# Strassen's scheme for the second product of both MLP layers, on weights split once and fetched back

## The reference, cut to what matters

```python
gate = 1.0 / (1.0 + np.exp(-(x @ w_gate)))      # layer 1, 512 -> 1536
x = (gate * (x @ w_val)) @ w_out                # 1536 -> 512
h = x @ w_in                                    # layer 2, 512 -> 2048
x = (h * (1.0 / (1.0 + np.exp(-1.702 * h)))) @ w_out2   # 2048 -> 512
```

## Time and profile before

| | us |
|---|---|
| median of 3 runs | 897.64 (897.04 to 898.20) |
| profiled execution, own time | 896.92 |
| its span | 895.2 |
| PE busy | 887.3 |
| POOL busy | 694.8 |
| ACT busy | 483.5 |
| DVE busy | 472.2 |
| granted TensorE clock | 1.000 |

### The profile page before, as it was taken

How to read it: one execution, slowest core, us unless ns; L and a number is a source line. 1 busy time by engine, 2 the same in 40 slices (tenths; PEclk the granted TensorE clock), 3 DMA queues, 4 the chain that set the end, 5 groups by cost and what they waited for, 6 DMA issues and landing times.

```text
span 895.2 us, 17338 instructions
## 1 busy us (share of the span) xinstructions
PE 887.3 (99%) x6572; PEld 831.2 (93%) x6572; DVE 472.2 (53%) x865; ACT 483.5 (54%) x967; POOL 694.8 (78%) x551
## 2 busy tenths in 40 slices
PE   8999999999999999999999999999999999999998
PEld 6878899999999999999898899999998999989897
DVE  5767545555555455554544455555545445454545
ACT  5777755554445455545555455544645554545542
POOL 6679989998779999758787869998757887566551
PEclk9999999999999999999999999999999999999999
DMA  9776112222221222222221222422222212132111
GB/s 333 251 226 219 54 62 71 71 69 74 69 67 55 71 72 71 71 71 71 71 71 52 67 72 70 141 72 71 71 72 68 74 48 93 50 120 92 48 48 70
DMA packets 26722, 80.38 MB, mean 90 GB/s; under 512 B 2960, under 2 KB 3216, under 8 KB 26640
## 3 DMA queue, kind: packets, MB, share of 16 engines
q1 hardware_dynamic: 26640, 79.28, 27.5%
HBM read 74.55 MB, written 4.72 MB: 89 GB/s over the span
## 4 chain that ended last, share of the span: by engine, by line
PE 98%; DMA 1%; SPq 1%; issue 0%; DVE 0%
PE o_ps L432 39%; PE d_ps L442 7%; PE d_ps L445 7%; PE d_ps L444 7%; PE s_ps L442 6%; PE s_ps L445 6%; PE s_ps L444 6%; PE t_ps L442 3%; PE t_ps L445 3%; PE t_ps L444 3%; PE o_ps L405 1%; PE o_ps L425 1%; PE t_ps L376 1%; PE t_ps L417 1%; PE s_ps L330 1%; PE t_ps L390 1%
## 5 line engine op out<-in xcount | busy, mean ns | idle before, releaser
L1271 DVE TENSOR_TENSOR att<-o_ps,att 128x512 f32<-128x512 f32 (+1 forms) x245 | 152.4, 626 | 150.5 <-PE o_ps L432 150.5
L1518 POOL TENSOR_TENSOR w_lo<-w_sum,w_hi 128x1024 fp32r<-128x1024 f32 x60 | 144.1, 2402 | 66.0 <-ACT w_hi L782 66.0
L1513 POOL TENSOR_TENSOR w_lo<-w_raw,w_hi 128x768 fp32r<-128x768 f32 x60 | 111.0, 1849 | 44.1 <-ACT w_hi L778 44.1
L442 PE MATMUL d_ps<-xs_hi,w_hi 128*128 128x384 f32 x360 | 120.5, 335 | 0.0
L445 PE MATMUL d_ps<-xs_hi,w_lo 128*128 128x384 f32 x360 | 120.4, 335 | 0.0
L444 PE MATMUL d_ps<-xs_lo,w_hi 128*128 128x384 f32 x360 | 120.4, 334 | 0.0
L1531 POOL TENSOR_TENSOR v_lo<-v_raw,v_hi 128x1024 fp32r<-128x1024 f32 x42 | 100.7, 2398 | 20.3 <-ACT v_hi L786 20.3
L432 PE MATMUL o_ps<-v_hi,g_hi 128*128 128x512 f32 x288 | 111.9, 389 | 0.8 <-DVE att L1271 0.8
L432 PE MATMUL o_ps<-v_hi,g_lo 128*128 128x512 f32 x288 | 112.3, 390 | 0.0
L432 PE MATMUL o_ps<-v_lo,g_hi 128*128 128x512 f32 x288 | 112.3, 390 | 0.0
L1492 POOL TENSOR_TENSOR w_sum<-w_raw 128x256 f32<-128x256 f32 x120 | 88.4, 736 | 23.6 <-PE t_ps L445 20.2
(11 more groups left out here) (135 smaller groups left out, 1993.6 us busy)
## 6 DMA issues: line engine op xcount, KB each, us to landing
v_raw<-in_w_out_dram SPq DMA_DIRECT2D x42, 512.0 KB, 3.5
w_raw<-in_w_gate_val_dram SPq DMA_DIRECT2D x36, 512.0 KB, 3.6
w_raw<-in_w_in_dram SPq DMA_DIRECT2D x24, 512.0 KB, 3.5
vw<-in_v_win_dram SPq DMA_DIRECT2D x16, 390.0 KB, 4.9
vt<-in_v_tok_dram SPq DMA_DIRECT2D x16, 320.0 KB, 3.8
qk<-in_q_t_dram SPq DMA_DIRECT2D x16, 288.0 KB, 3.5
qk<-in_k_t_dram SPq DMA_DIRECT2D x16, 288.0 KB, 4.5
out_dram<-att SPq DMA_DIRECT2D x17, 256.0 KB, 4.5
```

The lines of the kernel that those rows point to most:

```text
L442: pe.matmul(bank, wh[:, w, cols], xh[:, x, c, :], start=(start and c == 0), stop=False, skip_group_check=True)
L1271: vec.tensor_tensor(part, value, part, ALU.add).then_inc(y_added, 1)
L1513: gp.tensor_tensor(w_lo[b % 2][:, A11:A22 + 1, :], w_raw[b % 2][:, R11:R22 + 1, :], w_hi[b % 2][:, A11:A22 + 1, :], ALU.subtract).then_inc ...
L1518: gp.tensor_tensor(w_lo[b % 2][:, S1:S4 + 1, :], w_sum[b % 2][:, S1:S4 + 1, :], w_hi[b % 2][:, S1:S4 + 1, :], ALU.subtract).then_inc(ws_re ...
```

## The change

It changes all of the MLP but the first phase's group order and the arithmetic of the first product.

- Phases are (1,0), (1,1), (1,2), (2,0), (2,1), (2,2). Phase 0 keeps the plain second product. The other 36 groups go in 18 pairs c, c+1 (n is c+2, the next pair's first group). A pair's second product is Strassen's too, in both layers feature-major: 7 tiles of 2 outputs of 12 matmuls of 384 columns (`second_pair`, order in TILES). Activations get their own sums T1 to T4, made in PSUM by VectorE (make_t1 to make_t4), copied by ScalarE (save11, save21, save12, hi_t1 to hi_t4) and split.
- Output weights of a pair are split into 7 pieces by `split_pair` on GpSimd and v_a12 to v_a22 on ScalarE, 11 and 7 operations of 128x512. They have one buffer, whose slots come free as the tiles end (`v_free`). Their raw weights are loaded by `load_pair` into one buffer.
- Input weights are split once. Layer 1's twelve blocks are stored to DRAM in phase 0 (`spill`, 1.83 MB each), layer 2's eight are made as jobs 0 to 7 in phases 0 to 2 in unused x slots (`job_sums`, `job_lows`, `job_a`, `job_s`, `store_job`). From phase 1 on each block is fetched back in three transfers: five of seven pieces (1.31 MB) behind the fifth product of the block that had the slot (`fetch_12`), then one behind its sixth and one behind its seventh (`fetch_3`).
- x has 10 slots (`ring`) in place of 14: B11, B21, T2 of the next phase are made early, T1, T3, T4, B22 when the last block's products free their slots (`late_x`). With c+2 the first group of a phase, `late_x` stands on GpSimd ahead of `split_pair(c + 2)`.
- In layer 1's pairs ScalarE's list ends v_a12(n), hi_t4(d), v_s1(n), v_a11(n), the activations of n, v_s2(n), v_s4(n), v_s3(n). For the first pair v_a12, v_s1, v_a11 stand ahead of snap_u2 of the pair's last block and v_s2, v_s4, v_s3, v_a22 ahead of save11, hi11 and snap_u3. ScalarE's job_a and job_s stand ahead of snap_u2(FIRST[d]) or, for jobs 2, 4 and 7, of snap_u2(FIRST[n]).
- VectorE's list of pair_of_two ends: add 9, add 10, low11(n), add 11, c22(n), add 12, add 13, low22(n).
- The output leaves feature-major, one store per pass and eight of 192 KB at the end; the host transposes it.

The parts of the diff that the text speaks of (SP, PE, ACT, POOL in this order):

```diff
-OB1, OB2 = 2 * KC, 2 * NT // P
-PHASES = [(1, 0), (1, 1), (2, 0), (1, 2), (2, 1), (2, 2)]
+OB1 = 2 * KC
+PHASES = [(1, 0), (1, 1), (1, 2), (2, 0), (2, 1), (2, 2)]
...
+JOBS = G2
+JOB_AT = (7, 7, 4, 4, 4, 1, 1, 1)
+JOBS_BEFORE = (0, 2, 5, 8)
...
+TILES = ((VA12, B21, True, 0, 0), (VS1, T1, True, 1, 1), (VS4, B22, False, 0, 1), (VA11, B11, True, 0, 0),
+         (VS2, T2, False, 0, 1), (VS3, T3, False, 1, 1), (VA22, T4, False, 1, 0))
+OBP = 2 * NP
+SINCE = (8, 6, 10, 6, 4, 8, 14)
+G_OUT = {g: 2 * i + 2 for i, (v, g, start, r, t) in enumerate(TILES)}
+V_OUT = {v: 2 * i + 2 for i, (v, g, start, r, t) in enumerate(TILES)}
...
+def v_free(c, piece):
+    return y_count(c) if c == G1 else y_count(c - 2) + V_OUT[piece]
...
+            def fetch_12(b):
+                if b >= NB:
+                    return
+                if b < MADE + 2:
+                    sp.wait_ge(spilled[b % 2], 16 * (MADE // 2))
+                if b == FIRST[NL1]:
+                    sp.wait_ge(job_stored, 16 * JOBS)
+                sp.wait_ge(in_done[b % 2], count(b - 2, 5))
+                sp.dma_start(w[b % 2][:, :, A11:S3 + 1, :].bitcast(F32), w_split[split_at(b), :, :, A11:S3 + 1, :]).then_inc(w_in1[b % 2], 16)
+            def fetch_3(b):
+                if b >= NB:
+                    return
+                sp.wait_ge(in_done[b % 2], count(b - 2, 6))
+                sp.dma_start(w[b % 2][:, :, A22, :].bitcast(F32), w_split[split_at(b), :, :, A22, :]).then_inc(w_in3[b % 2], 16)
+                sp.wait_ge(in_done[b % 2], count(b - 2, 7))
+                sp.dma_start(w[b % 2][:, :, S4, :].bitcast(F32), w_split[split_at(b), :, :, S4, :]).then_inc(w_in4[b % 2], 16)
+            def load_pair(c):
+                if c >= NG:
+                    return
+                if c == G1:
+                    sp.wait_ge(wa_ready, MADE)
+                    sp.wait_ge(wsum_ready, MADE)
+                else:
+                    sp.wait_ge(vp_ready, NP * pair(c))
+                q, lay, p, g = GROUPS[c]
+                source = w_out1 if lay == 1 else w_out2
+                for i in range(2):
+                    sp.dma_start(raw[:, i, :, :].rearrange("p a n -> p (a n)"), source[g + i]).then_inc(vp_loaded, 16)
...
+            def store_job(j):
+                sp.wait_ge(job_lo, 2 * j + 2)
+                sp.dma_start(w_split[MADE + j], job_w[JOB_AT[j]][:, :, :, :].bitcast(F32)).then_inc(job_stored, 16)
...
+            for c in range(G1, NL1, 2):
+                steps = range(LAST[c] if c > G1 else FIRST[c + 1], FIRST[c + 2] + 1)
+                if c == G1:
+                    load_job(2)
+                if c == G1 + 6:
+                    load_job(5)
+                for b in steps:
+                    fetch_3(b + 1)
+                    fetch_12(b + 2)
+                    if b == FIRST[c + 1]:
+                        load_pair(c + 2)
+                    if c in (G1 + 2, G1 + 8) and b == FIRST[c + 1]:
+                        store_job(3 if c == G1 + 2 else 6)
+                        load_job(4 if c == G1 + 2 else 7)
+                if c in (G1, G1 + 6):
+                    store_job(2 if c == G1 else 5)
+                    load_job(3 if c == G1 else 6)
+                if c in (G1 + 2, G1 + 8):
+                    store_job(4 if c == G1 + 2 else 7)
+            for c in range(NL1, NG - 2, 2):
+                for b in (FIRST[c + 1], FIRST[c + 2]):
+                    fetch_3(b + 1)
+                    fetch_12(b + 2)
+                load_pair(c + 2)
...
+            def second_pair(c, i):
+                v_part, g_part, start, r, t = TILES[i]
+                pe.wait_ge(vp_ready, NP * pair(c) + V_LOWS[v_part])
+                if g_part in t_ready:
+                    pe.wait_ge(t_ready[g_part], strassen(c + 1))
                 else:
-                    s = o % (OB2 // 2)
-                    toks = slice(s * P, (s + 1) * P)
-                    passes(bank, [((gh[:, t, f, toks], gl[:, t, f, toks]), (vh[:, f, :], vl[:, f, :])) for f in range(FG)]
-                           ).then_inc(y_ready, 1)
+                    pe.wait_ge(g_ready[11 if g_part == B11 else 21 if g_part == B21 else 22], c + 2)
+                for j in range(2):
+                    n = y_count(c) + 2 * i + j
+                    pe.wait_ge(y_added, n - 1)
+                    cols = slice(j * P, (j + 1) * P)
+                    bank = o_ps[:, n % 2, 0:NT]
+                    for k in (c, c + 1):
+                        vh, vl = v_all[:, k % 2, 0, v_part, cols], v_all[:, k % 2, 1, v_part, cols]
+                        gh, gl = g_hi[k % 2][:, g_part, :], g_lo[k % 2][:, g_part, :]
+                        pe.matmul(bank, vh, gh, start=(start and k == c), stop=False, skip_group_check=True)
+                        pe.matmul(bank, vh, gl, start=False, stop=False, skip_group_check=True)
...
+            for c in range(G1, NL1, 2):
+                if c > G1:
+                    p4(FIRST[c])
+                    p3(FIRST[c])
+                    head(LAST[c])
+                step(FIRST[c + 1])
+                step(LAST[c + 1])
+                step(FIRST[c + 2])
+                for i in range(NP):
+                    second_pair(c, i)
+            for c in range(NL1, NG - 2, 2):
+                p4(FIRST[c])
+                p3(FIRST[c])
+                head(FIRST[c + 1])
+                step(FIRST[c + 2])
+                for i in range(NP if c + 4 < NG else NP - 2):
+                    second_pair(c, i)
+            c = NG - 2
...
+            def round_pair_s(c, v_part, n):
+                if c >= NG:
+                    return
+                act.wait_ge(vp_summed, 4 * pair(c) + n)
+                nc.scalar.copy(v_all[:, :, 0, v_part, :], v_f[:, :, 1, v_part, :]).then_inc(vp_hi, 1)
...
+            def pair_of_two(c):
+                d, n = c + 1, c + 2
+                q = GROUPS[c][0]
+                first, last = c == START[q], n == START[q + 1]
+                gelu21(c)
+                save21(c)
+                hi21(c)
+                gelu12(c)
+                snap_p1(FIRST[d])
+                save12(c)
+                gelu11(d)
+                snap_u2(FIRST[d])
+                hi_t1(c)
+                hi_t3(c)
+                save11(d)
+                hi11(d)
+                snap_u3(FIRST[d])
+                v_a22(c)
+                if last:
+                    round_t1(q + 1)
+                snap_p1(FIRST[n])
+                gelu22(d)
+                hi_t2(c)
+                gelu21(d)
+                save21(d)
+                hi21(d)
+                hi_t4(c)
+                hi22(d)
+                if last:
+                    round_t3(q + 1)
+                gelu12(d)
+                snap_u2(FIRST[n])
+                save12(d)
+                hi_t1(d)
+                snap_u3(FIRST[n])
+                hi_t3(d)
+                if first and q + 1 < len(PHASES):
+                    round_b11(q + 1)
+                    round_b21(q + 1)
+                hi_t2(d)
+                if c == START[q] + 2 and q + 1 < len(PHASES):
+                    round_t2(q + 1)
+                v_a12(n)
+                hi_t4(d)
+                gelu11(n)
+                if last:
+                    round_t4(q + 1)
+                    round_b22(q + 1)
+                v_s1(n)
+                v_a11(n)
+                save11(n)
+                hi11(n)
+                gelu22(n)
+                hi22(n)
+                v_s2(n)
+                v_s4(n)
+                if n + 2 < NG:
+                    v_s3(n)
...
+            def split_pair(c):
+                steps = 4 * pair(c)
+                pair_low(c, VA12, raw[:, :, V12, :])
+                pool.wait_ge(vp_loaded, 32 * pair(c) + 32)
+                pool.wait_ge(y_ready, v_free(c, VS1))
+                pair_sum(VS1, raw[:, :, V21, :], raw[:, :, V22, :], ALU.add)
+                pair_low(c, VA11, raw[:, :, V11, :])
+                pool.wait_ge(y_ready, v_free(c, VS2))
+                pool.wait_ge(vp_summed, steps + 1)
+                pair_sum(VS2, v_f[:, :, 1, VS1, :], raw[:, :, V11, :], ALU.subtract)
+                pool.wait_ge(vp_summed, steps + 2)
+                pair_sum(VS4, raw[:, :, V12, :], v_f[:, :, 1, VS2, :], ALU.subtract)
+                pair_low(c, VS1, v_f[:, :, 1, VS1, :])
+                pool.wait_ge(vp_summed, steps + 3)
+                pair_low(c, VS2, v_f[:, :, 1, VS2, :])
+                pair_low(c, VS4, v_f[:, :, 1, VS4, :])
+                pool.wait_ge(y_ready, v_free(c, VS3))
+                pair_sum(VS3, raw[:, :, V11, :], raw[:, :, V21, :], ALU.subtract)
+                pair_low(c, VS3, v_f[:, :, 1, VS3, :])
+                pair_low(c, VA22, raw[:, :, V22, :])
 
             def low_x(q, x, source, n):
                 pool.wait_ge(xhi_ready, NP * q + n)
...
+            for q in range(3, len(PHASES)):
+                for c in range(START[q], START[q + 1], 2):
+                    if q + 1 < len(PHASES):
```

(47 more changed lines are left out.)

1321 lines of the change are left out of this document (767 added, 554 removed).

## The result

The changed kernel takes 1058.54 us (median of 4 runs, 1056.24 to 1061.42) beside 897.92 for the kernel before (897.04 to 898.66): ratio 1.179, 95% interval 1.176 to 1.182. The profiled execution has a span of 1057.2 us.

What follows compares the result with a forecast made beforehand. TensorE's matmul count times spacing was taken as the bound. A floor of 862.3 us plus waits of 43 + 7 + 30 + 21 + 11 + 10 + 11 gave 995 us, forecast range 960 to 1030, 8-in-10 range 885 to 1030.

Steps and rivals of the forecast that it cites:

- The floor: Whole kernel: 896.9 us less 34.6 us of saved matmul time gives 862.3 us, if TensorE still waits for nothing.
- Sum of the stalls: All waits added to 862.3 us: 43 + 7 + 30 + 21 + 11 + 10 + 11.
- Step 1: Pair transitions: GpSimd's chain of weight sums delays snap_p1, so p6 waits 3.0 us in layer 2, 1.7 in layer 1.
- Step 2: Layer-2 transitions: raw weights land late behind the fetch; tiles wait 0.9 us, p6 4.5, together 5.4; eight cost 43.
- The rival with the loads in time: Loads and the jobs' stores are in time, only steps 1, 3, 4 and 6 count: 951 us; chance 0.21.
- Step 3: Four phase boundaries: late T1, T3, T4, B22 on GpSimd; 30 us for two in layer 2, 21 us in layer 1.
- Steps 4 and 5: First pair's v operations amid ScalarE's step work, 11 us; jobs 4 and 7 waiting for stores and loads, 10 us.
- The fetch of five: Five-piece fetch between steps: needs 5.3 of 7.1 us, costs nothing; rival that it binds, 1020 us, within the forecast's 0.56.

Runs made afterwards that it cites:

- e8: The kernel before with five extra ScalarE copies ahead of snap_p1 in 15 groups of phases (2,1) and (2,2): 924.9 us.
- e3: The changed kernel with ScalarE's v_s3 moved to stand ahead of v_a22 of the next pair, no longer ahead of its activations and snap_p1: 1004.7 us.
- e9: The changed kernel with hi_t4(d) ahead of v_a12(n) on ScalarE in both kinds of pair, nothing else: 1059.9 us.
- e2: The changed kernel with the pair's raw weights in layer 2 issued ahead of the last block's fetches, not behind them: 1022.2 us.
- e7: The kernel before with nine extra ScalarE copies ahead of snap_p1 in every second group of (2,1) and (2,2), 8 places: 934.9 us.

## Why the prediction was wrong

1058.5 us lies above 995 and above the range's 1030. The side, the two mechanisms and the sum of the waiting were right; a term was missing.

- **The floor (failed).** "862.3 us, if TensorE still waits for nothing", with every matmul at 0.1733, was added to the waits as if waiting left that spacing alone. The runs show 3.4 or 6.8 us at half clock at most waits of about 3 us, some 50 us lost in all. Without these the kernel would have taken some 1008 us, inside the range. The clock row is nines because that kernel has no wait of over 1 us in its MLP; a sum that adds 133 us of waits in pieces of 3 us can't keep it. The Trainium skill, "TensorE: Matmul & The Clock Gate", Terms, gives the penalty as the time throttled times one minus the clock's ratio. By this rule a stretch of 3.4 us would cost 1.7, an estimate; the traces nearly agree: with starts 0.32 instead of 0.1733 apart it costs 1.6. The losses of 50.2 and 11.2 us above are summed by the rule's form and confirm nothing by themselves.
- **Sum of the stalls: 133 predicted, 130.8 measured** as idle time. So close a sum is partly luck: the terms are off by up to 9 us both ways. The eight ordinary transitions in layer 2 took 49.5 us (43 predicted), the four in layer 1 6.5 (7), the boundaries 42.2 (51), the first pair 8.9 (11), the jobs 12.8 (10). Also missing were the ends and slower starts at each wait, 0.25 us per wait in e8.
- **Step 1, right.** p6 was to wait until T+7.2; the tiles of the transition shown end at 782.5, 4.2 ahead of the stop at 786.7, and p6 starts at 789.71, T+7.2. e3 removes it. GpSimd's 128x512 took 1.28 us, predicted 1.29, ScalarE's 0.62, predicted 0.60. Of the two rates that the prediction took from the Trainium skill, "GPSIMD Engine Reference", Performance versus the Vector engine, the best case is 0.77 us for 512 elements, and the measurement decides against it. The other, 2.6 cycles of 1.2 GHz, is 1.11, an estimate and also too low: the sum stood by the rows and not, as the prediction says, by this rate.
- **Step 2, right in size, not in its parts.** The pair was to land at TS+8.2 and came at about TS+9. Predicted: 0.9 us at the tiles and 4.5 at p6, 5.4 in all; measured 2.7 and 3.0, 5.7 in all. The step let v_a12 hold only v_a11, hi11 and low11; hi_t4(d) stands behind it too, with low_t4 and all additions from the sixth on. e9 takes that coupling away and finds 4.3 at p6, where 4.5 were predicted, and the same time. The rival with the loads in time was to be 44 us below the forecast; e2 is 36.3 below the change.
- **Step 3, somewhat too high.** 51 us for four boundaries; TensorE's waits there are 9.7 and 9.5 in layer 1 against 10.5 each, 10.4 and 12.6 in layer 2 against 15 each.
- **Steps 4 and 5, right in kind.** 11 and 10 us; measured 6.9 + 2.0 = 8.9, and 12.8.
- **The fetch of five** was said to need 5.3 of 7.1 us between steps. It lands after 6.4, and TensorE waited for it once, 0.2 us. It costs only by standing ahead of the raw pair.

## What to carry to other kernels

Where a change puts waits on a TensorE that had none, don't add them to a floor at full clock: in this kernel waits of 1.5 us cost themselves and 0.25 us, waits of 3 us mostly half as much again. One late transfer behind a large one, or one piece in the wrong place of an ordered list, is paid for at every iteration; look at what stands behind each new wait on its engine, list by list, and move that first (e2 and e3 are moved lines alone, and worth 97 us together). A scheme that saves 6% of the matmuls needs all the waits of a pair together, with what they cost beyond themselves, below that saving, here 1.84 us in 31.

## What had not been expected of the hardware

The same two waits did not cost the same in each pair. Two pairs of the change, each from raw load to raw load, each with the tiles' 2.7 and the snapshot's 3.0 us:

```profile
641.84:679.23 37.39, 31.60 (x170) 30.67 (x169) 21.79 (x43) 19.15 (x43) 15.79 (x12) 0.95 0.37 127
...
763.95:804.21 40.26, 34.45 (x170) 33.52 (x169) 21.78 (x43) 19.79 (x44) 21.19 (x15) 0.87 0.34 118
```

In the first, the clock fell at one of the waits, for 3.4 us; in the second at both, for 3.4 and 6.8 us, which is the 2.9 us more. And of e7's eight waits of 3.06 us, the one that ended at 693.40 was followed by none:

```profile
692.00:694.00 2.00, 0.60 (x4) 0.63 (x5) 0.00 (x0) 1.97 (x6) 1.92 (x3) 1.00 0.00 0
694.00:696.00 2.00, 2.00 (x13) 2.00 (x13) 1.03 (x2) 1.35 (x4) 0.83 (x2) 1.00 0.00 0
```

Over the twelve traces, from 120 us on, counting only waits with no other within 7 us before and 4 us behind, the clock fell at none of 60 under 1.7 us, at 7 of 16 from 1.7 to 2.1, at 32 of 47 from 2.6 to 3.15, and at all but two of 60 longer ones, mostly for 6.8 us where the wait was over 4.2. So length decides most, but not all. Short waits are not safe when they come close together: two of 1.4 and 1.8 us in the change, ending at 714.57 and 717.65, brought 6.8 us at half clock (717.4 to 724.2). What decides between two waits of the same length these runs don't show.
